# A fused attention, expert and feed-forward kernel: another order for the first attention units, a branch moved behind the first expert chunk, and one store moved behind a branch

## What is computed

```python
for t in range(S):                                  # S = 768, B = 4, H = 8, D = 48
    state = alpha[:, :, t, :, None] * state + np.einsum('bhd,bhe->bhde', k[:, :, t], v[:, :, t])
    y[:, :, t] = np.einsum('bhd,bhde->bhe', q[:, :, t], state)
...
expert_idx = np.argmax(logits, axis=1)              # logits = xn @ en.T / tau
h = np.maximum(x[mask] @ w1[e], 0.0)
out[mask] = gate_w[mask, None] * (h @ w2[e])
...
h = np.maximum(np.maximum(x @ w1, x @ w2), x @ w3)
return (h @ w_out)
```

## Time and profile before

| | us |
|---|---|
| median of 3 runs | 718.38 |
| lowest and highest | 717.15, 723.28 |
| the profiled execution's own time | 718.57 |
| its span (first to last instruction) | 716.9 |
| TensorE busy in it | 678.8 |
| VectorE, ScalarE, GpSimd busy | 305.6, 270.6, 337.5 |
| mean granted clock of TensorE | 0.98 |

### The profile page before, as it was taken

One profiled execution on the slowest core, in us unless ns is written; L12 is line 12 of the kernel. 1 busy time (PEld: TensorE's weight loads), 2 busy tenths in 40 slices (PEclk: granted clock), 3 DMA queues, 4 the chain that ended last, 5 costly groups with the idle time before them and its releaser, 6 DMA issues.

```text
span 716.9 us, 13419 instructions
## 1 busy us (share of the span) xinstructions
PE 678.8 (95%) x5268; PEld 609.3 (85%) x5269; DVE 305.6 (43%) x666; ACT 270.6 (38%) x586; POOL 337.5 (47%) x272
## 2 busy tenths in 40 slices
PE   5999999983999999999999999999999999999995
PEld 4888888872999999999999978888888888888885
DVE  7889997986712221212221344222223222233221
ACT  4788997863344444334342121111111111112110
POOL 5234444462487688687689247240430531410112
PEclk9999999995999999999999999999999999999998
DMA  9998995203563983452633142020020000000001
GB/s 186 208 205 187 221 202 154 85 20 106 197 223 91 271 311 123 159 194 79 224 75 103 38 148 74 12 77 30 24 95 0 22 22 11 22 12 0 23 23 44
DMA packets 130868, 77.08 MB, mean 108 GB/s; under 512 B 106000, under 2 KB 121128, under 8 KB 130800
## 3 DMA queue, kind: packets, MB, share of 16 engines
q1 hardware_dynamic: 121840, 61.08, 31.2%
q0 software_dynamic: 4032, 9.80, 3.6%
q10 hardware_dynamic: 4928, 5.29, 2.4%
HBM read 61.72 MB, written 14.44 MB: 106 GB/s over the span
## 4 chain that ended last, share of the span: by engine, by line
PE 77%; issue 14%; DVE 4%; POOL 3%; ACT 1%; POOLq 0%; ACTq 0%; DVEq 0%
PE bank L1658 44%; PE bank L1685 5%; PE bank L1686 5%; PE bank L1687 5%; PE bank L1425 4%; PE bank L1522 3%; PE bank L1463 3%; PE bank L1531 2%; PE bank L1473 2%; PE bank L1633 1%; PE bank L1510 1%; POOL out L661 1%; PE bank L1452 1%; DVE U L1023 0%; PE bank L1416 0%
## 5 line engine op out<-in xcount | busy, mean ns | idle before, releaser
L1658 PE MATMUL bank<-yh,mh 128*128 128x512 f32 x324 | 126.9, 392 | 0.9 <-ACT tm L944 0.9
L1658 PE MATMUL bank<-yh,ml 128*128 128x512 f32 x324 | 127.5, 394 | 0.0
L661 POOL DMA_INDIRECT out<-oo,ids x24 | 23.6, 985 | 197.1 <-DVE oo L1365 197.1
L602 POOL TENSOR_TENSOR wsp<-raw,wsp 128x1536 fp32r<-128x1536 f32 x28 | 97.6, 3511 | 22.3 <-ACT wsp L899 22.2
L1334 DVE SCALAR_TENSOR_TENSOR hTl<-bank,hTh 128x384 fp32r<-128x384 f32 (+4 forms) x64 | 36.9, 579 | 158.6 <-ACT hTh L881 158.3
L1658 PE MATMUL bank<-yl,mh 128*128 128x512 f32 x324 | 91.7, 391 | 0.0
L1658 PE MATMUL bank<-xh,wsp 128*128 128x384 f32 (+6 forms) x402 | 83.6, 343 | 1.0 <-ACT xh L919 1.0
L947 ACT CAST gh<-t 128x512 fp32r<-128x512 f32 x36 | 22.3, 620 | 151.4 <-DVE t L1376 151.4
L1658 PEld LDWEIGHTS bank<-yh,mh 128*128 128x128 f32 x324 | 60.9, 188 | 13.8 <-ACT tm L944 1.3
L1658 PEld LDWEIGHTS bank<-xh,wsp 128*128 128x128 f32 x402 | 70.4, 188 | 2.5 <-issue 1.4
L1658 PEld LDWEIGHTS bank<-yl,mh 128*128 128x128 f32 x324 | 60.8, 188 | 13.7
(11 more groups left out here) (258 smaller groups left out, 1229.1 us busy)
## 6 DMA issues: line engine op xcount, KB each, us to landing
raw<-in_moe_w SPq DMA_DIRECT2D x14, 1536.0 KB, 6.8
nat<-in_k SPq DMA_DIRECT2D x32, 144.0 KB, 3.2
nat<-in_q SPq DMA_DIRECT2D x32, 144.0 KB, 4.0
vt<-in_v SPq DMA_DIRECT2D x32, 144.0 KB, 3.1
attention_rows<-xc SPq DMA_DIRECT2D x4, 1152.0 KB, 6.9
yT_ff<-expert_columns SPq DMA_DIRECT2D x6, 768.0 KB, 4.4
nat<-in_alpha SPq DMA_DIRECT2D x30, 144.0 KB, 3.9
stg<-in_moe_w SPq DMA_DIRECT2D x3, 1152.0 KB, 18.3
```

What stands on the lines that cost most here:

```text
L602: g.tensor_tensor(wsp[:, to, 1, n, part], raw[:, n, part], wsp[:, to, 0, n, part].bitcast(f32), ALU.subtract).then_inc(w_lo[n], 1)
L661: g.indirect_dma_start(out=out, out_offset=bass.IndirectOffsetOnAxis(ap=ids[:, i, 0:1], axis=0), in_=oo[i % 2][:], in_offset=None).then_in ...
L1658: last = mm(o, x, y, start=(n == 0), stop=(n == len(todo) - 1))
```

## The change

The edits fall into four groups.

1. Attention's head on DVE: the six scans of unit 0 stand ahead of the norm of the expert embeddings; the scans of unit 1 behind the copies of the turned embeddings into `read`; the scans of unit 2 are cut in two calls of three, the first behind `scale_q(0, 0)`, the second behind the states of unit 0; `scale_q(1, 1)` stands ahead of the scans of unit 3.
2. Attention's head on ACT: `stage_a2(0, 0)` stands ahead of the copy of unit 1's alpha; `stage_a2(2, 2)` stands behind the carries of unit 0, not ahead of them.
3. PE ahead of the experts: the constant products are four instead of one and stand ahead of the wait for the flag; the first chunk stands ahead of the branch, once instead of once in each side. It is now called without the short program's arguments, so that the rows of the second chunk are turned at the full width of 432 and wait for all four gathers.
4. ACT: the flag is read before the first `If`; the store of the eighth chunk is taken out of that branch and stands in a second `If` on the same flag behind it.

```diff
--- before.py
+++ after.py
@@ -50,7 +50,7 @@
 NP_T = 2 * CH
 BT = 4
 NB = NT // BT
-WARM_X = 1
+WARM_X = 4
 LIMIT = 1e18
 CR = 8
 
@@ -796,7 +796,7 @@
         def step(u):
             b, j = u // UPB, u % UPB
             stage_c(u)
-            if u + 2 < NU:
+            if 0 < u < NU - 2:
                 stage_a2(u + 2, (j + 2) % UPB)
             carry(u, j, 0)
             if b and j:
@@ -804,6 +804,7 @@
             for c in range(1, CH - 1):
                 carry(u, j, c)
             if u == 0:
+                stage_a2(2, 2)
                 check_a(0, 0)
                 check_a(1, 1)
             if u + 2 < NU:
@@ -817,8 +818,8 @@
                 squares(b - 1, 2 * j - 1)
 
         stage_a(0, 0)
+        stage_a2(0, 0)
         stage_a(1, 1, 4)
-        stage_a2(0, 0)
         stage_a2(1, 1)
         stage_a(2, 2, 6)
         stage_a(3, 3, 4)
@@ -910,7 +911,8 @@
                 x_high(i + 1, k, after)
             if isinstance(i, int) and i == 0:
                 act.wait_ge(r_tab, 2)
-            y_out_of(i, n)
+            if more:
+                y_out_of(i, n)
 
         act.wait_ge(r_sqrt, 1)
         a.activation(es[:, 6:7], ident[0:E, 0:1], ACT.Exp)
@@ -921,7 +923,8 @@
         for turned, ks, cs in first_b:
             a.copy(xh[:, ks, cs], turned).then_inc(a_xh, ks.stop - ks.start)
         chunk(0, 0, 0)
-        with few_chunks(act):
+        few = act.value_load(few_t[0:1, 0:1], min_val=0, max_val=1)
+        with act.If(few > 0):
             for e in range(1, E):
                 chunk(e, e % 2, e if e < E - 1 else None, e < E - 1, WN[e], WN[(e + 1) % E])
         with act.Else():
@@ -935,6 +938,8 @@
             i = first_chunk(act, E - 1)
             chunk(i, 1)
             chunks_left(act, E - 1, i, 1, chunk)
+        with act.If(few > 0):
+            y_out_of(E - 1, WN[E - 1])
 
         def ff_block(bk, par, last=False):
             for f in range(KF2):
@@ -996,6 +1001,20 @@
         dve.wait_ge(ident_ready, 1)
         for jj in range(UPB):
             d.tensor_tensor(read[:, jj, 0:D], ident[:, 0:D], ident[:, HL:HL + D], ALU.add)
+        def scans(u, j, cs=range(CH)):
+
+            dve.wait_ge(act_a, 2 * u + (1 if cs[-1] < HC else 2))
+            if not (isinstance(u, int) and u < 4):
+                dve.wait_ge(act_UA, CR + 5 * (u - 3))
+            dve.wait_ge(act_sumA, CR + u - 3)
+            for c in cs:
+                last = d.tensor_tensor_scan(A[j][:, P * c:P * c + P], aT[j % 2][:, P * c:P * c + P],
+                                            floor[:], 1.0, ALU.mult, ALU.max)
+            if cs[-1] == CH - 1:
+                last.then_inc(dve_A, 1)
+
+        dve.wait_ge(const_ready, 1)
+        scans(0, 0)
         dve.wait_ge(e_act, 1)
         exact_norm(es[:, 1:2], es[:, 0:1], es[:, 4:5], es[:, 2:3], es[:, 3:4], unit=2.0 ** 12)
         link(d.reciprocal(es[:, 5:6], es[:, 4:5]))
@@ -1004,18 +1023,6 @@
         link(d.tensor_tensor(es[:, 5:6], es[:, 5:6], itau[0:E, :], ALU.mult))
         d.tensor_scalar(embp[:].rearrange("e (h d) -> e h d", d=HL)[:, :, 0:D],
                         embn[:].rearrange("e (h d) -> e h d", d=D), es[:, 5:6], None, ALU.mult).then_inc(e_dve, 1)
-        def scans(u, j):
-
-
-            dve.wait_ge(act_a, 2 * u + 2)
-            if not (isinstance(u, int) and u < 4):
-                dve.wait_ge(act_UA, CR + 5 * (u - 3))
-            dve.wait_ge(act_sumA, CR + u - 3)
-            for c in range(CH):
-                last = d.tensor_tensor_scan(A[j][:, P * c:P * c + P], aT[j % 2][:, P * c:P * c + P],
-                                            floor[:], 1.0, ALU.mult, ALU.max)
-            last.then_inc(dve_A, 1)
-
         def recip(u, j):
 
             dve.wait_ge(pool_u, CR + u + 1)
@@ -1099,6 +1106,8 @@
             for part in range(3):
                 mask(u, j, part)
             states(u, j)
+            if u == 0:
+                scans(2, 2, range(HC, CH))
             if u == NU - 3:
                 sum_logits(0, B - 1)
             if u == NU - 2:
@@ -1108,9 +1117,11 @@
                 link(d.tensor_scalar(fits[:], sums[:], LIMIT, None, ALU.is_lt))
                 d.tensor_reduce(good[:], fits[:].rearrange("p a u -> p (a u)"), AX.X, ALU.add).then_inc(fl_good, 1)
                 choose_early(link, r_run)
+            if u == 0:
+                scale_q(1, 1)
             if u + 3 < NU:
                 scans(u + 3, (j + 3) % UPB)
-            if u + 1 < NU:
+            if 0 < u < NU - 1:
                 scale_q(u + 1, (j + 1) % UPB)
             if u == NU - 2:
                 rank_early(link, r_rank, r_low)
@@ -1118,18 +1129,16 @@
                 recip(u + 2, (j + 2) % UPB)
                 scale_k(u + 2, (j + 2) % UPB)
 
-        dve.wait_ge(const_ready, 1)
-        scans(0, 0)
-        scans(1, 1)
         dve.wait_ge(e_pe, 1)
         for jj in range(UPB):
             last = d.tensor_copy(read[:, jj, D:D + E], bank[7][:, E * jj:E * jj + E])
         last.then_inc(e_copy, 1)
+        scans(1, 1)
         recip(0, 0)
         scale_k(0, 0)
         scale_q(0, 0)
+        scans(2, 2, range(HC))
         recip(1, 1)
-        scans(2, 2)
         scale_k(1, 1)
         for u in range(NU - UPB):
             step(u)
@@ -1715,11 +1724,12 @@
             down(KF - 1)
 
         pe.wait_ge(w0_lo, NU - UPB)
+        keep_warm(WARM_X, bank[3])
         pe.wait_ge(r_tab, 1)
         many = pe.value_load(many_t[0:1, 0:1], min_val=0, max_val=1)
+        lift_first(0)
+        chunk(0, 0, 0)
         with pe.If(many > 0):
-            lift_first(0)
-            chunk(0, 0, 0)
             pe.wait_ge(r_tab, 2)
             chunks_left(pe, 0, 0, 0, chunk)
             with pe.Fori(0, 3) as n:
@@ -1732,9 +1742,7 @@
             chunk(i, 1, E - 1)
             chunks_left(pe, E - 1, i, 1, chunk)
         with pe.Else():
-            keep_warm(WARM_X, bank[3])
-            lift_first(0)
-            for e in range(E):
+            for e in range(1, E):
                 chunk(e, e % 2, e, e < E - 1, WN[e], WN[(e + 1) % E], True)
 
         def out_product(bk, par, t, dst):
```

## The result

| | before | after |
|---|---|---|
| median, us | 718.38 | 723.13 |
| lowest and highest | 717.15, 723.28 | 721.77, 725.10 |
| the profiled execution's own time | 718.57 | 723.62 |
| its span | 716.9 | 721.9 |

A forecast was written before the change was run, and what follows sets the result against it. The prediction took PE as the bound, busy 678.8 of 716.9 us. 718.6 + 2.9 (head) - 4.0 (ahead of the experts) + 5.6 (branch) - 0.9 (end) = 722.2, or 722.0 from the median; range 715 to 727.5.

The forecast's parts named there:

- The head: Start of attention: the reordering on DVE and ACT plus a clock fall on PE cost +2.9 us, bounds -1.3 and +3.5.
- 10.5 + 0.85 + 2.0 = 13.5. Unit 0 gains about 0.7: Attention's head on DVE: unit 1's scans wait for an alpha copy and end at 13.5; unit 0 gains about 0.7 us.
- the 1.2 of the forecast: Attention's head: ACT's passes of unit 2, now behind the carries, make `turn_kp(1)` start at 29.3, a loss of 1.2 us.
- The clock term: Attention's head: PE's clock falls behind a pause of nearly 4 us and slows the following work, taken as 1.7 us.
- A second one in the earlier burst: Attention's train: a rival with a second PE pause in the burst at m = 8, +3.6 us, 725.6; chance 0.08.
- Ahead of the experts: From router to first expert product on PE: without the jump, the first product comes 4.0 us earlier, bounds -5 and -2.
- if the clock again rises 4.7 after the start: Constant products ahead of the experts: PE's clock rises at 173.1, so the four products end at 173.3.
- The branch: PE between chunks 0 and 1: code fetch 3.9 plus low clock 1.7, together +5.6 us, bounds 0 and +10.
- a quarter of a microsecond at most: Chunk 1 on PE: the cost claimed for turning its rows at the wider width.
- The rival in which the branch is free: Between chunks 0 and 1: PE decides the branch ahead of time and continues without a gap, 716.4 us; chance 0.20.
- the code queue behind weights for 8: Between chunks 0 and 1: rival, code page queues behind weights, branch costs 8 + 1.7 us, total 726.1; chance 0.15.
- The end: From experts to feed-forward: ACT jumps while PE still multiplies, so PE's wait goes; gain 0.9 us, bounds 0 and -0.9.

The follow-up runs named there:

- a4: The changed kernel without PE's branch: the long program left out, chunks 1 to 7 follow chunk 0 directly; 718.57 us, ratio to before 1.0013.
- b1: The kernel before with group 4 alone (ACT reads the flag early, eighth chunk's store in a second If); 715.41 us, ratio to before 0.9980.
- a1: The changed kernel with groups 1 and 2 (attention's head) taken back, groups 3 and 4 kept; 716.93 us, ratio to before 0.9987.
- a2: The changed kernel with group 3 taken back: one constant product, and the first chunk inside both sides of the branch; 722.65 us, ratio to before 1.0070.
- a3: The changed kernel with five unused constant products filling PE's pause in the head, ahead of the turned k of unit 2; 720.37 us, ratio to before 1.0033.
- b2: The kernel before with only the head's early part: scans of units 0 and 1 and unit 0's passes moved; 719.93 us, ratio to before 1.0039.
- d2: The changed kernel with the six loads of the first expert's weights one step later in SP's list; 722.53 us, ratio to before 1.0074.
- b4: The changed kernel with chunk 0 called with the short program's arguments, so chunk 1's rows are turned at 384 columns; 722.28 us, ratio to before 1.0074.
- e: The changed kernel with POOL's products of units 0 and 2 held until the scans of units 1 and 3 are done; 725.49 us, ratio to before 1.0128.
- best: The kernel before with four constant products ahead of PE's wait for the flag, branch left in place, plus group 4; 712.78 us, ratio to before 0.9942.
- b3: The kernel before with only the four constant products moved ahead of PE's wait for the flag, first chunk left in the branch; 714.38 us, ratio 0.9961.
- d1: The kernel before with the six loads of the first expert's weights one step later in SP's list; 716.97 us, ratio to before 0.9995.

## Why the prediction was right, and where it was not

**The place of the losses and gains was right.** Of the marks named: PE paused between chunk 0 and chunk 1 with a low clock behind; no wait for ACT near 414; the passes of unit 2 stood behind the second half of its scans, and `turn_kp(1)` moved with ACT's copy of alpha 4. a4 and b1 showed by time that the branch costs and the store gives (4.0 and 1.4; forecast 5.6 and 0.9), and a1 that the head loses. That the sum came within 1.1 us is in part luck. By the medians the head costs 5.9 and the rest of the change gives 1.1 (a1), where the forecast had 2.9 and a further loss of 0.7; and a2 finds no loss in PE's part, where 1.6 was forecast. Each of these differences has an interval of about 2 us.

**The head was sized too small: +4.35 for +2.9.** The step that failed is "10.5 + 0.85 + 2.0 = 13.5. Unit 0 gains about 0.7" (the sum itself is 13.35), and with it that the masks of unit 0 "begin at about 19.4". Each duration was taken from a row in which the scans had no product of POOL beside them, and the change moved them under these products. Unit 1's scans took 2.84 and ended at 14.1; the first three of unit 2 took 1.91 and not 1.0. So the masks began at 20.58, and the other three scans of unit 2, which took their 1.05, ended at 24.43 and not at 23.4. The passes of unit 2 began at 24.47, and this 1.05 came through to `turn_kp(1)`. With the 1.2 of the forecast that makes 2.25, what a3 leaves for the order. b2 shows the early part alone on before: 1.08.

**The clock term was close: 2.10 for 1.7.** a3 gives it directly, for the profiled execution; counted in the same way from `turn_k(2)`, it is 1.6 in d2's and 2.9 in those of a4 and b4. The forecast set it behind `turn_kp(1)`; 0.54 of it came ahead, since `turn_k(2)` ran at half clock too (1.51 for 0.84). Together with the 1.05 this is why `turn_kp(1)` came at 30.85 and not at 29.3.

**The pauses: one rival partly came.** "A second one in the earlier burst" did appear, in unit 6. It did so in all eight traces whose `turn_kp(1)` is at 29.1 or later (after, a2, a3, a4, b2, b4, d2, e; 0.56 to 2.27 us), and with the old head only in best (0.54), not in before, a1, b1, b3 or d1. In after its price was not 3.6: the clock held, and the unit was 1.7 longer. In a3 and a4 the full price did come: the clock fell, and unit 6 took 12.81 and 12.75. In after's profile the pause of unit 10 shrank from 3.6 to 1.7 in all. That left +0.18 where 0 was forecast. The prediction's reading of the pause, program code arriving late, is borne out by the packets. Unit 10's pause differs between executions (absent in a1, a3 and b3), so one profile does not fix its mean: by the medians the head's whole cost is 5.9 (a1), by the marks 4.35. The other 1.5 is within the interval; the pause in unit 6, and the longer low clock of a4 and b4, are candidates for it.

**Ahead of the experts, -3.67 for -4.0**, with an error inside: "if the clock again rises 4.7 after the start" put the rise at 173.1 plus the head's loss of 4.5, 177.6. It came at about 178, 5.2 behind the start at 172.80, so all eight rows ran at half clock and ended at 178.23. The 4.7 was one execution's: in the others with these products the rise came 2.8 (a3, b4) to 5.8 (a4) behind their start, and the stretch took 8.5 to 9.6. The gain itself does not hang on the branch: b3 has 2.8 of it without moving it.

**The branch: +5.4 for +5.6 plus the turn's 0.25.** The branch itself was sized too dear, 4.2 for 5.6: the pause was 2.70 idle (2.9 against a4) and not 3.9, the low clock 1.33 and not 1.7. The 3.9 came from a branch for which PE still had to load the flag: in the kernel before its packet of code starts 1.5 behind PE's last product (159.93 against 158.43), here 0.2 behind it (see the last section). What filled the gap is the term waved through as "a quarter of a microsecond at most": the wider turn of chunk 1 costs 1.16 by a4 and 1.2 by b4. The rival in which the branch is free did not come; nor did the code queue behind weights for 8, though the DMA share was 0.87 in the window 215 to 216. The Trainium skill (Runtime: NRT & Kernel Launch, Instruction fetch mechanics) states that a taken branch to code outside the window at hand must fetch it by DMA before execution goes on. The traces agree: a packet of code runs from 213.49 to 214.46, 0.20 behind PE's last product, PE goes on at 215.99, and in a4 the pause is gone with the branch.

**The end: -1.2 for -0.9.** PE's wait of 0.94 is gone, and by b1 group 4 gives 1.4 [0.5, 2.4].

The errors had opposite signs only in part: head +1.45, turn and branch -0.2, warm products +0.3, end -0.3, the train +0.2, together +1.4, which is the distance from 3.6 to 5.0.

## What to carry to other kernels

Before an instruction is moved, look at what runs on the other engines at its new place: a DVE instruction with two SBUF inputs that starts under a GpSimd product of two SBUF tiles pays up to the whole rest of that product, and holding the product back, tried once here (e), moved the wait to the next such DVE instruction and cost more. A branch is cheapest where its engine waits anyhow: put idle-time work ahead of the jump and leave the jump there, rather than moving it between two stages that ran without a gap. When a pause is called "issue", look in the DMA records for a packet of program code that ends just ahead of its end. In a train that is full on one engine, put nothing behind the last wait of its head that had been done in a hole before.

## What the runs showed of the hardware that was not expected

**DVE behind GpSimd.** A scan of 128 columns takes 0.39 us alone and took 1.88 when it began 0.22 behind the start of a GpSimd product of 1.81; the reciprocal's correction went from 0.93 to 2.55. GpSimd's own product did not get longer in these cases (1.81), in which it had started first; where the reciprocal had, it took 2.37.

**Pauses and the clock.** The pause between chunks 0 and 1 was in six profiles at different lengths. Behind 2.26 (b4), 2.57 (a1) and 2.63 (e) the granted clock stayed at 1.00; behind 2.70 (after and a3) and 3.05 (d2) it fell to 0.50. In attention it fell behind 1.67 (before), 1.84 (b2), 2.25 (a4) and 2.27 (a3), and held behind 1.39 and 1.43 (after), 1.70 and 2.26 (b4) and 2.00 (e). A pause alone therefore doesn't say whether the clock falls. What the fall costs at chunk 1, from its first product to the feed-forward stage, is 1.3 in after, 1.9 in a3 and 2.8 in d2; in the head it is 2.1 by a3.

The windows of e and after at chunk 1's start show the two cases:

```profile
218.00:219.00 1.00, 1.00 (x7) 1.00 (x7) 0.00 (x0) 0.00 (x0) 0.83 (x1) 1.00 0.69 252
```

It has seven products in a microsecond at clock 1.00, where after has four at 0.50.

**A jump has two prices, and the fetch is in both.** With the flag just written, PE goes on 4.7 after it: 2.2 until the packet of code starts at 171.95, 1.0 for the packet, 1.5 from its end to the first product. With the flag read long before, it is 2.3 to 3.1 after PE's last product; in after 0.2, 1.0 and 1.5. In b3 the packet (168.25 to 169.19) ran beside the last constant products, and PE's idle time fell to 1.58.
